# Gate weights multiplied into the out weights on the chip, and the logits taken as 16 more columns of the out product

## What is computed

```python
x  = attention(q, k, v, mem_k, mem_v)      # windows: 32 queries, 16 left, 8 right, 8 memory keys; 8 heads of 64
h  = x @ w_in                              # 512 -> 1024
e  = np.exp(h - max(h));  sm = e / (sum(e) + 1e-9)
u  = h * sm
ln = (u - mean(u)) / np.sqrt(var(u) + 1e-6) * g_ln
x2 = ln @ w_out                            # 1024 -> 512
logits = x2 @ w_gate                       # 512 -> 8, picks the expert (argmax) and its weight (softmax)
eom    = 1 / (1 + np.exp(-(x2 @ w_output_gate)))   # 512 -> 8
out[token] = gate_w * eom[e] * (np.maximum(x2 @ w1[e], 0) @ w2[e])
```

## Time and profile before

| what | us |
|---|---|
| median of 3 runs (834.62 to 836.08) | 836.05 |
| span of the profiled execution, first to last instruction | 830.3 |
| TensorE busy | 795.2 |
| VectorE busy | 442.7 |
| ScalarE busy | 318.3 |
| POOL busy | 189.0 |

### The profile page before, as it was taken

The page is one execution under the profiler, slowest core; times in us unless marked ns, Lnnn a source line. Parts: engine busy times, 40 slices in busy tenths (PEclk is TensorE's granted clock), DMA queues, the critical chain, the costliest instruction groups (busy, mean ns, idle before and its releaser), DMA issues.

```text
span 830.3 us, 14051 instructions
## 1 busy us (share of the span) xinstructions
PE 795.2 (96%) x4416; PEld 681.5 (82%) x4417; DVE 442.7 (53%) x665; ACT 318.3 (38%) x425; POOL 189.0 (23%) x350
## 2 busy tenths in 40 slices
PE   4799999999999999999999799999999999999994
PEld 4688888888888888888877588888888888888883
DVE  4766665666665666666673771622444353644121
ACT  3544344443444443434333252512334353433210
POOL 4121343343311211111211221211221221221121
PEclk9999999999999999999999999999999999999998
DMA  9522333434222322223102561331163433421100
GB/s 295 185 77 82 123 102 113 145 120 126 76 76 97 128 78 76 76 76 117 47 13 63 204 229 54 138 124 49 43 231 122 148 134 129 169 99 36 37 25 20
DMA packets 22776, 88.89 MB, mean 107 GB/s; under 512 B 4062, under 2 KB 4190, under 8 KB 20960
## 3 DMA queue, kind: packets, MB, share of 16 engines
q1 hardware_dynamic: 16800, 71.80, 24.5%
q0 software_dynamic: 5952, 16.79, 6.4%
HBM read 77.82 MB, written 13.89 MB: 110 GB/s over the span
## 4 chain that ended last, share of the span: by engine, by line
PE 93%; DVE 3%; DMA 1%; issue 1%; ACT 1%; SPq 0%; POOL 0%; POOLq 0%; DVEq 0%; ACTq 0%
PE banks L1057 70%; PE banks L1083 5%; PE banks L1067 4%; PE banks L1201 3%; PE banks L1074 3%; PE banks L1101 2%; PE banks L1127 2%; PE banks L1178 2%; PE banks L1121 1%; DMA stage<-w_both 1%; DVE xT_lo L808 0%; ACT xT_hi L596 0%; DVE place_hot L871 0%; DVE he L788 0%; DVE ssum L769 0%
## 5 line engine op out<-in xcount | busy, mean ns | idle before, releaser
L1057 PE MATMUL banks<-slots_hi_lo,rT_hi 128*128 128x512 f32 x464 | 149.5, 403 | 0.2 <-issue 0.2
L1057 PE MATMUL banks<-slots_hi_lo,xsT_hi 128*128 128x512 f32 x464 | 124.4, 390 | 0.3 <-issue 0.3
L1057 PEld LDWEIGHTS banks<-slots_hi_lo,xsT_hi 128*128 128x128 f32 x464 | 86.8, 188 | 18.3 <-issue 0.5
L1057 PEld LDWEIGHTS banks<-slots_hi_lo,rT_hi 128*128 128x128 f32 x464 | 83.8, 190 | 15.3 <-issue 0.3
L1057 PE MATMUL banks<-slots_hi_lo,rT_lo 128*128 128x512 f32 x232 | 91.5, 394 | 0.0
L534 POOL DMA_INDIRECT out<-ys,rows_out x29 | 29.6, 1021 | 246.9 <-DVE ys L1028 246.9
L653 ACT ACTIVATE r_sb<-banks 128x1024 f32<-128x1024 f32 x29 | 29.7, 1026 | 132.2 <-PE banks L1057 132.2
L1057 PE MATMUL banks<-wout_hi,uT_hi 128*128 128x512 f32 x192 | 77.4, 403 | 0.8 <-DVE uT_lo L777 0.8
L1021 DVE TENSOR_TENSOR slots_hi_lo<-raw_w,slots_hi_lo 128x1024 fp32r<-128x1024 f32 x56 | 65.0, 1223 | 22.4 <-ACT slots_hi_lo L703 22.4
L1057 PE MATMUL banks<-wout_hi,uT_lo 128*128 128x512 f32 x192 | 75.2, 392 | 0.0
L910 DVE TENSOR_TENSOR rT_lo<-banks,rT_hi 128x1024 fp32r<-128x1024 f32 x29 | 35.5, 1225 | 74.3 <-ACT rT_hi L659 74.3
(11 more groups left out here) (175 smaller groups left out, 1412.3 us busy)
## 6 DMA issues: line engine op xcount, KB each, us to landing
raw_w<-experts SPq DMA_DIRECT2D x14, 2048.0 KB, 7.3
q_sb<-q_t SPq DMA_DIRECT2D x24, 512.0 KB, 3.7
k_sb<-k_win SPq DMA_DIRECT2D x24, 384.0 KB, 4.4
v_sb<-v_win SPq DMA_DIRECT2D x24, 384.0 KB, 5.1
x_rows<-x SPq DMA_DIRECT2D x24, 256.0 KB, 2.1
stage<-experts POOLq DMA_DIRECT2D x8, 512.0 KB, 3.8
stage<-w_both SPq DMA_DIRECT2D x4, 512.0 KB, 7.7
he<-w_both SPq DMA_DIRECT2D x1, 512.0 KB, 9.9
```

Source lines behind the costliest of these rows:

```text
L1057: ins = mm(o, lhs, rhs(part, k, n), start=(k == first and lhs is not None and part == 0 and parts == (0, 1)), stop=(k == final and parts = ...
```

## The change

The product of `w_out` with the 16 columns of both gates is made once on the chip: a transposed copy of `w_out` (2 MB) is loaded as a further input, `fold_gates` multiplies it with the gates (32 matmuls of 16 columns, 64 passes, placed after the input product of block 0), VectorE multiplies with `g_ln`, ScalarE and VectorE split the result in its high and low part behind the columns of `wout_hi` and `wout_lo`, whose rows of 512 columns become rows of 528. The out product of a block writes 528 columns as two halves of 264 in banks 4 and 5, so each chunk takes 6 matmuls in place of 3. `scale_y` reads both halves; the last 16 columns of x2 in SBUF are the logits, which `copy_logits` takes from there. `x2_turn`, `gate_logits` and `copy_x2T` are gone, with the tile `x2T` and their semaphores. `score_ps` moves to banks 6 and 7.

```diff
+YW = DM + 2 * E
+YB = YW // 2
...
+        wout_t = nc.alloc_sbuf_tensor_at("wout_t", [P, KD * DF], F32, offset=slot0)
+        gate_fold = nc.alloc_sbuf_tensor_at("gate_fold", [P, KF, 2 * E], F32, offset=slot0 + KD * DF * 4)
...
-            wout_hi = ra.take("wout_hi", [P, KF * DM], F32R)
-            wout_lo = ra.take("wout_lo", [P, KF * DM], F32R)
+            wout_hi = ra.take("wout_hi", [P, KF * YW], F32R)
+            wout_lo = ra.take("wout_lo", [P, KF * YW], F32R)
...
-        score_ps = bank(5, 2)
+        y2_ps = [bank(n)[:, 0:YB] for n in (4, 5)]
+        y_both = bank(4, 2).rearrange("p (b n) -> p b n", n=BANK)[:, :, 0:YB]
+        fold_ps = bank(5)[:, 0:KF * 2 * E]
+        score_ps = bank(6, 2)
...
             load_weights(range(4, EW // CH))
+            sp.dma_start(wout_t[:, :], wout_t_in).then_inc(wout_t_s, 16)
             load_qk(At(0, 2))
...
-                at_least(act, x2T_ps_s, b.i - 1)
-                nc.scalar.activation(x2[b.par][:, :], y_ps, ACT.Copy, scale=rstd[:, b.par:b.par + 1]).then_inc(x2_s, 1)
-
-            def copy_x2T(b):
-                act.wait_ge(x2T_ps_s, b.i + 1)
-                at_least(act, log_s, b.i)
-                nc.scalar.activation(x2T[:, :], gate_ps, ACT.Copy).then_inc(x2T_s, 1)
+                at_least(act, logc_s, b.i - 1)
+                nc.scalar.activation(x2[b.par][:, :].rearrange("p (h n) -> p h n", h=2), y_both, ACT.Copy,
+                                     scale=rstd[:, b.par:b.par + 1]).then_inc(x2_s, 1)
+
+            def high_fold():
+                act.wait_ge(fold_s, 1)
+                nc.scalar.activation(wout_hi[:, :].rearrange("p (k n) -> p k n", n=YW)[:, :, DM:YW], gate_fold[:, :, :],
+                                     ACT.Copy).then_inc(fold_hi_s, 1)
...
             square_u(At(0, 0))
+            high_fold()
             walk_a(act, step)
...
+            def scale_fold():
+                dve.wait_ge(fold_ps_s, 1)
+                nc.vector.tensor_tensor(gate_fold[:, :, :], fold_ps.rearrange("p (k n) -> p k n", n=2 * E),
+                                        wide(g_col[:, :], 2 * E), ALU.mult).then_inc(fold_s, 1)
+
+            def low_fold():
+                dve.wait_ge(fold_hi_s, 1)
...
             def copy_logits(b):
-                dve.wait_ge(log_s, b.i + 1)
+                dve.wait_ge(x2_s, b.i + 1)
                 nc.vector.tensor_copy(logits[:, bass.ds(b.i, 1), :].rearrange("p o n -> p (o n)"),
-                                      gate_ps[:, 0:2 * E]).then_inc(logc_s, 1)
+                                      x2[b.par][:, DM:YW]).then_inc(logc_s, 1)
...
             solu(At(0, 0))
+            scale_fold()
+            low_fold()
             walk_a(dve, step)
...
-                last = split_product([y_ps], lambda k: uT_hi[:, k * P:(k + 1) * P], lambda k: uT_lo[:, k * P:(k + 1) * P],
-                                     lambda part, k, n: (wout_hi, wout_lo)[part][:, k * DM:(k + 1) * DM],
+                last = split_product(y2_ps, lambda k: uT_hi[:, k * P:(k + 1) * P], lambda k: uT_lo[:, k * P:(k + 1) * P],
+                                     lambda part, k, n: (wout_hi, wout_lo)[part][:, k * YW + n * YB:k * YW + (n + 1) * YB],
...
+            def fold_gates():
+
+                pe.wait_ge(wout_t_s, 16)
+                pe.wait_ge(late_in_s, 32)
+                for k in range(KF):
+                    for d in range(KD):
+                        last = mm(fold_ps[:, k * 2 * E:(k + 1) * 2 * E], wout_t[:, d * DF + k * P:d * DF + (k + 1) * P],
+                                  gates_w[:, d * 2 * E:(d + 1) * 2 * E], start=(d == 0), stop=(d == KD - 1))
+                last.then_inc(fold_ps_s, 1)
...
             def step(s):
-                a, b, c, d = s + 1, s, s + -1, s + -2
+                a, b, c = s + 1, s, s + -1
                 scores(a)
-                if d.within(NBLK):
-                    gate_logits(d)
                 product_in(b, range(0, 1))
...
                 attention(a)
-                x2_turn(c)
...
             product_in(At(0, 0), range(KD // 2, KD))
+            fold_gates()
             walk_a(pe, step)
             ranks(0, EARLY)
             last_b = At(0, NBLK - 1)
-            gate_logits(last_b + -2)
...
             u_turn(last_b)
-            x2_turn(last_b + -1)
-            gate_logits(last_b + -1)
             product_out(last_b, range(0, KF // 2))
             xs_turn(At(0, 0))
             product_out(last_b, range(KF // 2, KF))
-            hidden(At(0, 0), range(0, 1))
-            x2_turn(last_b)
-            hidden(At(0, 0), range(1, 2))
-            gate_logits(last_b)
-
-
-            hidden(At(0, 0), range(2, KD - 1))
+            hidden(At(0, 0), range(0, KD - 1))
             ranks_late()
```

More of the change, by code:

```diff
@@ L81, in at_least, with build @@
     eng.wait_ge(sem, value)
-def build(nc, q_in, k_in, v_in, w_in, g_in, gates_in, experts_in, const_in, const_bf_in, x2_dram, out):
+def build(nc, q_in, k_in, v_in, w_in, wout_t_in, g_in, gates_in, experts_in, const_in, const_bf_in, x2_dram, out):
     with ExitStack() as ctx:
@@ L172, in build @@
         x2_at = ra.at
-        x2 = [ra.take(f"x2_{n}", [P, DM], F32) for n in range(2)]
-        x2T = ra.take("x2T", [P, DM], F32)
+        x2 = [ra.take(f"x2_{n}", [P, YW], F32) for n in range(2)]
         stage_at = ra.at
@@ L241, in build @@
         y_ps = bank(4)
-        score_ps = bank(5, 2)
+        y2_ps = [bank(n)[:, 0:YB] for n in (4, 5)]
+        y_both = bank(4, 2).rearrange("p (b n) -> p b n", n=BANK)[:, :, 0:YB]
+        fold_ps = bank(5)[:, 0:KF * 2 * E]
+        score_ps = bank(6, 2)
         gate_ps = bank(7)
-        first_ps = bank(5)[:, BANK // 2:BANK // 2 + 2]
-        rank_ps, tot_ps = (bank(n)[:, 0:NBLK * E].rearrange("p (i e) -> p i e", e=E) for n in (5, 6))
+        first_ps = bank(6)[:, BANK // 2:BANK // 2 + 2]
+        rank_ps, tot_ps = (bank(n)[:, 0:NBLK * E].rearrange("p (i e) -> p i e", e=E) for n in (6, 7))
         tile_gate_ps = bank(6)[:, BANK // 2:BANK // 2 + 3 * NTILE]
@@ L292, in build @@
         x2_s = sem("x2_ready")
-        x2T_ps_s = sem("x2_transposed")
-        x2T_s = sem("x2T_copied")
         late_in_s = sem("gain_and_gates_loaded")
-        log_s = sem("logits_done")
+        wout_t_s = sem("w_out_transposed_loaded")
+        fold_ps_s = sem("gates_times_w_out_done")
+        fold_s = sem("gates_times_w_out_scaled")
+        fold_hi_s = sem("folded_gates_high_split")
+        fold_lo_s = sem("folded_gates_low_split")
         logc_s = sem("logits_copied")
@@ L575, in high_weights @@
                             k = 2 * (c - W1C // CH) + m
-                            last = nc.scalar.activation(wout_hi[:, k * DM:(k + 1) * DM],
+                            last = nc.scalar.activation(wout_hi[:, k * YW:k * YW + DM],
                                                         stage[STAGE[c]][:, m * DM:(m + 1) * DM],
@@ L641, in step @@
                 high_x(s + 1)
-                copy_x2T(s + -1)
                 square_u(s)
@@ L679, in _ @@
             high_u(last)
-            copy_x2T(last + -1)
             xt(At(0, 0))
             scale_y(last)
-            copy_x2T(last)
             relu(At(0, 0))
@@ L737, in low_weights @@
                         last = nc.vector.scalar_tensor_tensor(
[L738 to L739 removed]
+                            wout_lo[:, k * YW:k * YW + DM], stage[STAGE[c]][:, m * DM:(m + 1) * DM],
+                            g_col[:, k:k + 1], wout_hi[:, k * YW:k * YW + DM].bitcast(F32),
                             ALU.mult, ALU.subtract)
@@ L812, in low_x @@
                 last.then_inc(xlo_s, 1)
+            def scale_fold():
[4 more added lines that the diff above has]
+                dve.wait_ge(fold_hi_s, 1)
+                by_k = "p (k n) -> p k n"
+                nc.vector.tensor_tensor(wout_lo[:, :].rearrange(by_k, n=YW)[:, :, DM:YW], gate_fold[:, :, :],
+                                        wout_hi[:, :].rearrange(by_k, n=YW)[:, :, DM:YW].bitcast(F32),
+                                        ALU.subtract).then_inc(fold_lo_s, 1)
             def copy_logits(b):
-                dve.wait_ge(log_s, b.i + 1)
+                dve.wait_ge(x2_s, b.i + 1)
                 nc.vector.tensor_copy(logits[:, bass.ds(b.i, 1), :].rearrange("p o n -> p (o n)"),
-                                      gate_ps[:, 0:2 * E]).then_inc(logc_s, 1)
+                                      x2[b.par][:, DM:YW]).then_inc(logc_s, 1)
             def step(s):
@@ L1106, in product_out @@
                     pe.wait_ge(wout_lo_s, (EW - W1C) // CH)
-                    pe.wait_ge(late_in_s, 32)
+                    pe.wait_ge(fold_lo_s, 1)
                 if 0 in chunks:
@@ L1115, in product_out @@
                     last.then_inc(y_s, 1)
-            def x2_turn(b):
-                pe.wait_ge(x2_s, b.i + 1)
-                at_least(pe, logc_s, b.i)
-                for k in range(KD):
```

(15 more changed lines are left out.)

6 lines of the change are left out of this document (2 added, 4 removed).

## The result

The change makes the kernel slower: 849.74 us median of 4 runs (848.81 to 853.1) against 835.34 us (831.69 to 836.08) on the same chip, ratio 1.0187 with a 95% interval of 1.0161 to 1.0212, or +14.4 us. The forecast was 842.9 with a range up to 848.5. The sign was right, the size was less than half of what came.

The account below looks back on a forecast made before the run. TensorE, busy 96% of the span, was taken as the bound. Start +2.7, 22 steps of +0.22 (+4.9) and end -0.8 gave +6.8 us on the 830.3 us span; with 5.75 us to the median, 842.9 us, range 835.5 to 848.5.

Parts of the forecast that it names:

- The sign: Whole kernel: the change was forecast to make it slower, chance 0.75.
- The wait that replaces the saving: Before each input product: TensorE waits 1.11 us for x's low part, keeping 0.17 of 1.28 us saved per step.
- The narrow matmuls: Out product: 48 matmuls of 264 columns at 0.122 us replace 24 of 512, adding 0.39 us per block.
- Rival (a): Out product: the weight load sets the narrow matmuls' pace; at 0.110 us each, 829.6 us in total; chance 0.12.
- The step: Each of 22 loop steps: 0.39 - 0.17 = +0.22 us, period 17.86 us, +4.9 us in all.
- The start: Fold after block 0's input product: 7.0 us of work, partly filling idle time, clock staying at 2.4 GHz; +2.7 us.
- Rival (b): Fold: the clock falls; half the fold costs 3.3 us, the input product after up to 1.6; 846 to 848 us; chance 0.22.
- The end of the phase: Last blocks up to the late ranks: x2T waits go, other waits come, last block's work removed; -0.8 us.
- Both replacement waits: End of the phase: the x2T waits (2.4 us) give way to waits for low parts of block 23's x and u.
- rival d: Loop: the new waits of 1.11 us per step lower the clock; total far over 860 us; chance 0.02.
- The base: Whole kernel: the median of 836.05 lies 5.75 us above the profiled span of 830.3, a difference kept in the forecast.
- What cost nothing: Transposed w_out's load lands about 30 us, just in time; ScalarE's wider copy of y and the logits copy add nothing.

Follow-up runs that it names:

- e4: Changed kernel with the out product's last two chunks issued behind attention and ScalarE's copy of x ahead of its copy of y: 833.72 us, ratio 0.9984.
- e7: e4 with TensorE transposing the probabilities one chunk earlier and ScalarE copying them before the exponential of h: 827.21 us, ratio 0.9914.
- e6: Kernel before with the rows of wout_hi and wout_lo at a pitch of 528 columns, 512 used: 837.36 us, ratio 1.0035.
- e3: Kernel before plus the load of transposed w_out, the 64 thin passes and their scaling, results unused: 842.62 us, ratio 1.0085.
- e5: Changed kernel with the fold turned round: gates stationary, w_out moving, 16 passes of 512 columns in place of 64 of 16: 848.48 us, ratio 1.0170.
- e1: Changed kernel with 896 bytes left free ahead of the staging region, giving the token tiles their old SBUF offset: 847.79 us, ratio 1.0153.
- e10: Changed kernel in its own order with the edits of e1 and e5 together: 843.51 us, ratio 1.0118 to before.
- e11: Changed kernel once more with no edit, as a control on the chip of e10 and e8: 851.56 us, ratio 1.0208.
- e2: Kernel before with its staging region beginning 128 bytes later: 838.64 us, ratio 1.0056.
- e8: e7 with the edits of e1 and e5 added: 819.91 us, ratio 0.9831 to before.
- e12: e9 with GpSimd writing expert 0's low part by a copy in place of a subtraction: 860.31 us, ratio 1.0301.
- e9: Changed kernel with four x2 transposes and eight 16-column passes per block put behind attention, results unused: 872.06 us, ratio 1.0456.

## Why the prediction was right and wrong

**The wait that replaces the saving: right.** 1.11 us per step was taken; the waits show 0.95 us on the matmul row and 1.11 on its weight load. The total of 24.3 us meets the forecast's "some 24 us" partly by luck: 21 waits of 0.95 us are 20, and the rest is one of 1.75 us at the start (1.4 in before) and the one of 2.56 us in front of block 23. e4 and e7 show that this wait was what ate the saving: with it covered the step is 16.86 us against 16.75 by the sum of the work. Both runs change the order on TensorE and on ScalarE at once, so the part of each is not shown.

**The narrow matmuls: right.** 0.122 us was taken. The chain has 18 matmuls of 512 and 24 of 264 columns in 7.04 us and 24 of 264 in 2.93, which is 0.122 each. By the rule of the Trainium skill (TensorE: Matmul & The Clock Gate, "Back-to-back issue gap") they would take 0.1125; the trace disagrees at this width too. Rival (a) is out. e6 puts a part of the 0.39 us per block on the pitch, which the prediction had put wholly on the width; that does not touch the sum.

**The step: right.** +0.22 was forecast (period 17.86), +0.246 measured (17.88).

**The start: wrong, and this is the main failed step.** The words were: "With TensorE never idle I expect 2.4 GHz to stay". TensorE was never idle there and the clock was 0.50 for 10.2 us. Rival (b), with 0.22, happened, and at its price: it had +3.3 us for the fold and up to 1.6 behind it; the fold took 10.14 - 7.04 = 3.1 more and the scores 3.41 - 1.76 = 1.65 more. The start came to +9.1 - 1.1 = +8.0 in place of +2.7. The row against it was a stretch of 3.90 us with some thin passes in it; the fold is 7 us of nothing else. The prediction also read the first scores, 16 passes in 3.73 us, as a case of half clock. The trace of before has its first clock record at 26.2 us, so it does not show the clock of those scores; after's scores behind the fold do bear the price out, 3.71 us at 0.50. e3 measured the term alone, +8.0 on the median, and e5 showed by a dense form of the same products that the excess over the work was the clock. The 7.0 us of work itself were costed right.

**The end of the phase: its clock was left out.** -0.8 was forecast, and the two profiled executions show +2.5. Both replacement waits were foreseen (2.56 and 2.37 us), but costed only as time. 10.2 us of half clock stand beside them, of which half, some 5 us, is the loss; with those off, the stretch would be shorter than before, as forecast. The prediction asked of new waits only whether they lower the clock within the steady loop (rival d: they did not, 1.00 through the step). But the +2.5 holds for these two executions and not for the kernels. From block 23's input product to the late ranks the changed kernel's end took 31.47 us in after, 30.16 in e1, 30.06 in e5, 30.15 in e10 and 28.72 in e11, with 10.2, 6.8, 6.8, 6.8 and 3.4 us of half clock; the end of before took 28.93, 29.52 in e2, 28.92 in e3 and 31.51 in e6, with none, 3.4, none and 6.8. The means differ by +0.4 us, so the sign of this term is not shown. Nor is it shown what lowers the clock there. It fell beside the first wait in all five profiles that have its 2.56 us, and beside the second in four of them. Of the five profiles in which the first wait is only 1.1 to 1.3 us and the second has its 2.37, e7, e8 and e12 have no half clock before the late ranks, e4 has 3.4 us and e9 6.8. And it fell in e2 and e6 too, which have neither wait, only those for x2T of 1.3 and 1.0 us. So the first wait at its full length has half clock beside it each time, shorter waits only in some executions.

**The tiles: missed altogether.** Nothing in the prediction looks behind the phase that the change edits. e1 and e2 give +4.0 us for it by address alone. With the start and this term right, the sum would have been 6.8 + 5.3 + 4.0 = 16.1 against +14.4 measured, and +17.9 in e11.

**The base.** 5.75 us were kept between span and median; 1.8 of them lie around the span, and the rest is that the profiled execution was quicker than the median. That did not hurt the forecast, which was a difference. Two small slips stand in the numbers: the upper 0.1244 us gives 845.6 us and not 845, and the sum of +6.8 moves the late ranks by 6.8 us and not 6. The profile has them 17.1 us later.

**What cost nothing: right.** The load of `wout_t` landed 10.4 us after its issue at 17.46, at 27.9 us, 9 us ahead of the fold. It took longer than the 7.3 us named as its bound, and landed in time all the same. The wider copy on ScalarE and the copy of the logits appear in no wait.

The +1.4 us of the first 37 us was not forecast and is not the change's: the same multiply of VectorE takes 2.82 us at 16.89 in after, beside GpSimd's split of `win_lo`, and 0.96 in before. It takes 2.8 to 3.1 us in ten of the fourteen profiles of this study, among them all three variants of before (e2, e3, e6), and 0.96 in three variants of after (e7, e8, e12).

## What to carry to other kernels

Before a piece of TensorE work is taken out, ask which input of the next piece it was covering; the saving is the slack of that input and no more, until other work is moved into the hole, and then the next chain (here the probabilities) has to be brought forward with it. Cost a run of narrow matmuls, and the work behind it, at half clock unless a row shows such a run of that length at full clock; the orientation with a wide moving side did the same work in the same time without the fall. Compare the offsets and pitches of buffers that an edit moves without meaning to, before giving a difference of half a per cent to what it computes.

## What was not expected of the hardware

- A matmul of 512 columns follows the last by 8.18 / 36 = 0.2272 us or 8.32 / 36 = 0.2311 us by where buffers lie in SBUF; 128 bytes change it (e2), 896 change it back (e1), 1024 leave it (e6).
- 16-column passes, back to back with no idle time, brought the granted clock from 1.00 to 0.50 in all eight profiles that have them, after 3.7 us of them in after and 4.6 in e3; the same products with 512 moving columns did not in all three that have those (e5, e8, e10; in e5 7.0 us at 1.00).
- A pass of 512 columns of plain f32 took 0.44 us (e5), one of the type that the split products use 0.23.
- VectorE's multiply of two tiles in SBUF ended 0.81 to 0.83 us behind the GpSimd instruction that had started before it, whether that took 2.37 us with two inputs (e9) or 1.04 with one (e12). In before the order at the start is the other way round: the multiply starts at 17.33 and takes 0.96 us, and GpSimd's split, at 17.36, takes 3.15 us in place of 2.34.
